# GpSimd issues its own transfers of the split w1 batches, and x is split straight from PSUM, in a three-stage fp32 kernel

## What is computed

```python
for t in range(S):                                   # linear attention with decay
    cur = einsum('bhd,bhe->bhde', u[None] * kt, vt)
    y[:, :, t] = einsum('bhd,bhde->bhe', rt, state + cur)
    state = wt[:, :, :, None] * state + einsum('bhd,bhe->bhde', kt, vt)
x = (((x @ w1) * (x @ w2)) @ w3) @ w_out             # gated layer
logits = x @ w_gate; P = exp(logits - logits.max())  # routing, 8 rounds of
for _ in range(8):                                   # normalising rows and columns
    P /= P.sum(1, keepdims=True) + 1e-09
    P /= P.sum(0, keepdims=True) + 1e-09
    P *= N / E
for e in range(E):                                   # every expert on every token
    out += P[:, e:e + 1] * (np.maximum(x @ w1[e], 0.0) @ w2[e])
```

## Time and profile before

| | |
|---|---|
| median of 3 runs | 2145.22 us (2140.44 to 2147.58) |
| the profiled execution's own time | 2151.62 us |
| its span in the profile | 2149.8 us |
| TensorE busy | 2043.4 us, 95% |
| VectorE, ScalarE, GpSimd busy | 1194.3, 816.0, 698.5 us |
| mean granted TensorE clock | 0.982 of full |
| moved by transfers | 314.92 MB, 146 GB/s over the span |

### The profile page before, as it was taken

How to read it: one execution, slowest core, us unless ns; L and a number is a source line. 1 busy time by engine, 2 the same in 40 slices (tenths; PEclk the granted TensorE clock), 3 DMA queues, 4 the chain that set the end, 5 groups by cost and what they waited for, 6 DMA issues and landing times.

```text
span 2149.8 us, 40177 instructions
## 1 busy us (share of the span) xinstructions
PE 2043.4 (95%) x16048; PEld 1695.3 (79%) x16048; DVE 1194.3 (56%) x1879; ACT 816.0 (38%) x1472; POOL 698.5 (32%) x892
## 2 busy tenths in 40 slices
PE   7799999999989789999999999999999999999998
PEld 4599889889867667777877888878877888878877
DVE  3567766675556345555575554454556445545544
ACT  4455555554433223333343333333334333333332
POOL 2566756673454764110142111011124101111111
PEclk9899999999999989999999999999999999999999
DMA  8544334431156666445454354444443444444442
GB/s 201 126 122 126 116 104 120 120 108 58 39 200 202 220 215 221 161 166 182 166 168 134 133 166 146 151 153 141 147 139 113 167 144 153 160 140 148 139 140 103
DMA packets 139529, 314.92 MB, mean 146 GB/s; under 512 B 11921, under 2 KB 77649, under 8 KB 139345
## 3 DMA queue, kind: packets, MB, share of 16 engines
q1 hardware_dynamic: 138656, 311.89, 44.7%
q10 hardware_dynamic: 688, 0.48, 0.1%
HBM read 239.87 MB, written 71.27 MB: 145 GB/s over the span
## 4 chain that ended last, share of the span: by engine, by line
PE 38%; issue 21%; POOL 2%; DVE 2%; DMA 1%; POOLq 0%; ACT 0%; SPq 0%; DVEq 0%; ACTq 0%
PE ps L1526 13%; PE ps L1528 13%; PE ps L1527 13%; POOL x L741 2%; DVE h_lo L1263 0%; DVE xs_lo L1078 0%; DMA late<-w_rows 0%; DMA Pb<-p_rows 0%; DMA w_raw<-w 0%; POOL x L779 0%; DVE tmp L1276 0%; DVE tb L1254 0%; PE ps L1620 0%; DVE tb L1258 0%; POOLq L92 0%
## 5 line engine op out<-in xcount | busy, mean ns | idle before, releaser
L741 POOL TENSOR_TENSOR x<-x,tmp 128x512 f32<-128x512 f32 x126 | 168.9, 1361 | 953.4 <-DVE tmp L1276 941.4
L1528 PE MATMUL ps<-h_hi,w 128*128 128x512 f32 x1152 | 457.6, 397 | 0.0
L1526 PE MATMUL ps<-h_hi,w 128*128 128x512 f32 x1152 | 456.6, 396 | 0.0
L1527 PE MATMUL ps<-h_lo,w 128*128 128x512 f32 x1152 | 456.5, 396 | 0.0
L819 ACT ACTIVATE tb<-ps 128x512 f32<-128x512 f32 x378 | 226.2, 598 | 509.5 <-PE ps L1528 486.6
L1014 ACT ACTIVATE h_hi<-tb 128x512 fp32r<-128x512 f32 x378 | 238.7, 632 | 451.3 <-DVE tb L1258 232.9
L1254 DVE TENSOR_TENSOR tb<-tb,ps 128x512 f32<-128x512 f32 x252 | 172.5, 686 | 289.2 <-PE ps L1528 283.4
L1263 DVE SCALAR_TENSOR_TENSOR h_lo<-tb,h_hi 128x512 fp32r<-128x512 f32 x378 | 289.3, 766 | 41.8 <-ACT h_hi L1014 35.5
L1258 DVE TENSOR_TENSOR tb<-ps,tb 128x512 f32<-128x512 f32 x252 | 173.9, 691 | 242.2 <-PE ps L1528 241.1
L1527 PEld LDWEIGHTS ps<-h_lo,w 128*128 128x128 f32 x1152 | 218.8, 190 | 51.7
L1526 PEld LDWEIGHTS ps<-h_hi,w 128*128 128x128 f32 x1152 | 217.8, 189 | 51.0
(11 more groups left out here) (154 smaller groups left out, 3181.2 us busy)
## 6 DMA issues: line engine op xcount, KB each, us to landing
early<-w_rows SPq DMA_DIRECT2D x63, 1024.0 KB, 5.6
late<-w_rows SPq DMA_DIRECT2D x63, 896.0 KB, 5.2
w<-w_rows SPq DMA_DIRECT2D x128, 384.0 KB, 4.3
w_rows<-batch SPq DMA_DIRECT2D x105, 384.0 KB, 3.2
w_rows<-w SPq DMA_DIRECT2D x64, 384.0 KB, 2.8
w_raw<-w SPq DMA_DIRECT2D x32, 576.0 KB, 4.8
Pb<-p_rows SPq DMA_DIRECT2D x24, 512.0 KB, 6.1
K<-kT SPq DMA_DIRECT2D x24, 192.0 KB, 3.7
```

The costliest lines, as they stand in the source:

```text
L741: return gp.tensor_tensor(to, a, b, ALU.add)
L1526: mm(o, w_hi, x_hi, start=start, stop=False, skip_group_check=True)
L1527: mm(o, w_hi, x_lo, start=False, stop=False, skip_group_check=True)
L1528: return mm(o, w_lo, x_hi, start=False, stop=stop, skip_group_check=True)
```

## The change

- GpSimd issues the batches' stores itself, behind each batch, and the load of the next raw w1 behind the fifth one (`make_batch`, new `load_w1` in GpSimd's program). SyncE's `keep_batch` and `load_w1` are gone, and so are SyncE's waits on `w1_made`.
- Batches begin in unit 2 (FROM_UNIT) and there are five to a unit, so 50 are made in the units. The other 55 go to the groups: four to a group, three where the y's of a later expert are added, two in group 5; the last two in group 16. In GpSimd's program of a group one batch stands ahead of the steps S4 to S6, and the others behind them.
- `xT` and GpSimd's `take_x` are gone. In slot 3 ScalarE copies all 128 rows from PSUM straight into the high plane of `yT` (256 columns) and of `x0` or `x1` (768 columns), in one instruction each where there were two. In slot 5 (was slot 6) VectorE subtracts both from PSUM into the low planes (`split_last_y`, `take_x`). Only then may SyncE issue the six moves, which carry both planes, 32 KB each. `go_up` waits for the moves (`gap_moved`) instead of for `x_split`.
- `load_early(0)`, GpSimd's and ScalarE's start on the third stage now wait for one more slice of the last unit (`up_done`, 89 instead of 88).
- The buffers of the batches are placed at the end of SBUF.

```diff
-    PER_UNIT = 6
+    FROM_UNIT, PER_UNIT = 2, 5
...
-        x_hi1 = sb("x_hi1", [P, KD, CT], f32r)
-        x_lo1 = sb("x_lo1", [P, KD, CT], f32r)
+        x1 = sb("x1", [P, 2, KD, CT], f32r)
...
-        x_hi = [sb("x_hi0", [P, KD, CT], f32r), x_hi1]
-        x_lo = [sb("x_lo0", [P, KD, CT], f32r), x_lo1]
+        x01 = [sb("x0", [P, 2, KD, CT], f32r), x1]
...
-        yT = sb("yT", [P, CT])
-        xT = sb("xT", [P, KD, CT])
...
+        yT = sb("yT", [P, 2, CT], f32r)
...
-        BEFORE = PER_UNIT * (U - 1)
-        in_unit = lambda u: range(PER_UNIT * (u - 1), PER_UNIT * u)
-        in_group = lambda G: range(min(LAST_BATCH, BEFORE + BATCHES * (G - 1)), min(LAST_BATCH, BEFORE + BATCHES * G))
+        BEFORE = PER_UNIT * (U - FROM_UNIT)
+        in_unit = lambda u: range(PER_UNIT * (u - FROM_UNIT), PER_UNIT * (u + 1 - FROM_UNIT)) if FROM_UNIT <= u < U else range(0)
...
+        per_group = lambda G: 0 if G == 0 else 2 if G == P_TURN[0] + 1 else 3 if any(y_at[n] and y_at[n][0] == G for n in range(6, Y)) else 4
+        made_before = [min(LAST_BATCH, BEFORE + sum(per_group(i) for i in range(G))) for G in range(NG + 1)]
+        in_group = lambda G: range(made_before[G], made_before[G + 1]) if G < NG else range(0)
+        assert all(BATCHES * G <= made_before[G] for G in range(1, NG))
...
-                        sp.dma_start(xT[HROW * h + HD:HROW * h + HROW, k, :],
-                                     yT[HROW * h + GAP * k:HROW * h + GAP * k + GAP, :]).then_inc(gap_moved, 16)
...
-            def load_w1(n):
-                if n:
-                    sp.wait_ge(w1_made, BATCHES * n)
-                for i, j, e, f in pieces(full_at(n)):
-                    sp.dma_start(w1_raw[:, KD * i:KD * j, :].rearrange("p (f k) c -> p f (k c)", k=KD),
-                                 w12[e, :, f:f + j - i, 0:D]).then_inc(w1_loaded, 16)
-
-            def keep_batch(x):
-                n, j = divmod(x, BATCHES)
-                sp.wait_ge(w1_made, x + 1)
-                sp.dma_start(w1_rows[n, :, :, BATCH * j:BATCH * j + BATCH, :], batch[x % 2][:, :, :, :].bitcast(f32)).then_inc(w1_kept[x % 2], 16)
-                if j == BATCHES - 1 and n + 1 < NG - 1:
-                    load_w1(n + 1)
+                        sp.dma_start(x01[u % 2][HROW * h + HD:HROW * h + HROW, :, k, :].bitcast(f32),
+                                     yT[HROW * h + GAP * k:HROW * h + GAP * k + GAP, :, :].bitcast(f32)).then_inc(gap_moved, 16)
...
-            load_w1(0)
...
-                for x in made[0:2]:
-                    keep_batch(x)
-                if u + 1 < U:
...
-                sp.wait_ge(y_copied, 2 * u)
+                sp.wait_ge(y_split, u)
+                sp.wait_ge(x_split, u)
...
-                for x in made[4:]:
-                    keep_batch(x)
...
-            sp.wait_ge(up_done, NF * (U - 1))
+            sp.wait_ge(up_done, NF * (U - 1) + 1)
...
-                made = in_group(G) if g else ()
-                for x in made[0:2]:
-                    keep_batch(x)
...
-                            for x in made[2:]:
-                                keep_batch(x)
...
-            def take_x(u):
-                pool.wait_ge(x_copied, 2 * u + 2)
-                pool.wait_ge(gap_moved, GAP_MOVE * (u + 1))
-                if u >= 2:
-                    pool.wait_ge(up_done, NF * (u - 1))
-                gp.tensor_copy(x_hi[u % 2][:, :, :], xT[:, :, :]).then_inc(x_hi_made, 1)
-                pool.wait_ge(x_hi_made, u + 1)
...
+            def load_w1(n):
+                for i, j, e, f in pieces(full_at(n)):
+                    gp.dma_start(w1_raw[:, KD * i:KD * j, :].rearrange("p (f k) c -> p f (k c)", k=KD),
+                                 w12[e, :, f:f + j - i, 0:D]).then_inc(w1_loaded, 16)
...
-            for u in range(U + 1):
-                if 1 <= u < U:
-                    for x in in_unit(u):
-                        make_batch(x)
+                gp.dma_start(w1_rows[n, :, :, BATCH * j:BATCH * j + BATCH, :], batch[x % 2][:, :, :, :].bitcast(f32)).then_inc(w1_kept[x % 2], 16)
+                if j == BATCHES - 1 and n + 1 < NG - 1:
+                    load_w1(n + 1)
+
+            for u in range(U):
+                if u == FROM_UNIT - 1:
+                    load_w1(0)
+                for x in in_unit(u):
+                    make_batch(x)
                 if u + 1 < U:
                     begin_rpad(u + 1)
-                if u:
-                    take_x(u - 1)
-                if u < U:
-                    copy_blocks(u)
-            pool.wait_ge(x_split, U)
-            pool.wait_ge(up_done, NF * (U - 1))
+                copy_blocks(u)
...
+                add_ys(S1, S4)
...
+                for x in made[0:1]:
...
-                add_ys(S3, R2)
-                for x in made[2:]:
+                add_ys(S4, R3)
+                for x in made[1:]:
                     make_batch(x)
-                add_ys(R2, NP)
...
-                for h in range(2):
-                    rows = slice(HROW * h, HROW * h + HD)
-                    copy(yT[rows, :], y_ps[rows, CT * LAST:CT * PAIRS]).then_inc(y_copied, 1)
-
-            def copy_y(u, h):
+                copy(yT[:, 0, :], y_ps[:, CT * LAST:CT * PAIRS]).then_inc(y_copied, 1)
+
+            def copy_y(u):
                 act.wait_ge(y_made, 2 * u + 2)
-                if u:
-                    act.wait_ge(x_split, u)
-                rows = slice(HROW * h, HROW * h + HD)
-                copy(xT[rows, :, :], y_ps[rows, 0:CT * LAST].rearrange("p (g t) -> p g t", t=CT)).then_inc(x_copied, 1)
+                if u >= 2:
+                    act.wait_ge(up_done, NF * (u - 1))
+                copy(x01[u % 2][:, 0, :, :], y_ps[:, 0:CT * LAST].rearrange("p (g t) -> p g t", t=CT)).then_inc(x_copied, 1)
...
-                        copy_y(u - 1, 0)
-                    if k == 4:
-                        copy_y(u - 1, 1)
+                        copy_y(u - 1)
...
-                    act.wait_ge(x_split, U)
-                    act.wait_ge(up_done, NF * (U - 1))
+                    act.wait_ge(up_done, NF * (U - 1) + 1)
...
+            def split_last_y(u):
+                dve.wait_ge(y_copied, u + 1)
+                dve.wait_ge(x_copied, u + 1)
+                low_part(yT[:, 1, :], y_ps[:, CT * LAST:CT * PAIRS], yT[:, 0, :]).then_inc(y_split, 1)
+
             def take_x(u):
-                dve.wait_ge(x_hi_made, u + 1)
-                low_part(x_lo[u % 2][:, :, :], xT[:, :, :], x_hi[u % 2][:, :, :]).then_inc(x_split, 1)
+                x = x01[u % 2]
+                low_part(x[:, 1, :, :], y_ps[:, 0:CT * LAST].rearrange("p (g t) -> p g t", t=CT), x[:, 0, :, :]).then_inc(x_split, 1)
...
-                if 1 <= u <= U and k == 6:
+                if 1 <= u <= U and k == 5:
+                    split_last_y(u - 1)
                     take_x(u - 1)
...
-                    pe.wait_ge(x_copied, 2 * u)
+                    pe.wait_ge(x_split, u)
...
-                    pe.wait_ge(x_split, u + 1)
+                    pe.wait_ge(gap_moved, GAP_MOVE * (u + 1))
...
-                                             x_hi[u % 2][:, k, :], x_lo[u % 2][:, k, :], k == 0, k == KD - 1)
+                                             x01[u % 2][:, 0, k, :], x01[u % 2][:, 1, k, :], k == 0, k == KD - 1)
...
-                    pe.wait_ge(x_copied, 2 * U)
+                    pe.wait_ge(x_split, U)
```

21 lines of the change are left out of this document (9 added, 12 removed).

## The result

The changed kernel takes 2084.99 us (median of 4 runs, 2082.86 to 2087.58) against 2146.4 us for the kernel before (the three runs told of above and a fourth): ratio 0.972, 95% interval 0.969 to 0.974, so some 61 us faster. The forecast was 2110 us and its range ended at 2087, so the gain was under-estimated.

A forecast was written before the change was run, and what follows sets the result against it. TensorE, busy for 95% of the span, was taken as the bound, so only its idle time and clock could be won. -41 + 12 - 6 = -35 us from 2145.2 gave 2110 us, range 2087 to 2137.

The forecast's parts named there:

- the circle: Groups 1 to 8: GpSimd waits for transfers that SyncE issues late, standing 147.0 us for GpSimd's batches.
- Part 1: Groups 1 to 8: SyncE no longer waits for batches; 28 us of waits and 13 of clock go, -41 us.
- the 4 us that I kept for `early` behind P: Groups 1 to 8: 4.0 of TensorE's 32.1 us of waits stay, as SyncE still waits for the turned P.
- Part 2: Groups 1 to 16: GpSimd pays for its transfers, TensorE held 10 us, clock 2 us: +12 us; units nothing.
- The price: GpSimd's time for issuing one transfer, taken at 1.1 us, between bounds of 0.52 and 3.7 us.
- The factor of two: GpSimd needs 829 ns for what VectorE does in 423, so an issue costs twice SyncE's 0.52 us.
- Part 3: Units: x's new path only moves TensorE's idle time, 17 us in all; 6 us of clock gained: -6 us.
- A: GpSimd quick enough, 0.6 us an issue, nothing held: 2098 us, or 2090 with moves landing within 2 us; chance 0.22.
- B: Units: path of x longer, each wait 3.5 us instead of 1.4: 2158 us, at half of that 2134; chance 0.09.
- C: Groups: GpSimd becomes the bound at 2.0 us an issue and the kernel slower: 2160 us; chance 0.10.
- D: SyncE stays blocked elsewhere (turned P, w2's split, products), perhaps 15 us won: 2130 us; chance 0.05.
- The signs: What the profile after should show in groups and units: waits, clock, group lengths, issues at 1.1 us.

The follow-up runs named there:

- sync_moves: The changed kernel with the transfers of w1's batches back on SyncE; new plan and new path of x stay: 2142.3 us, ratio 0.998.
- queue_alone: The kernel before with only w1's transfers issued by GpSimd; old plan of batches and old path of x stay: 2152.0 us, ratio 1.001.
- even_plan: The changed kernel with three batches in each group (two in group 5) where most had four: 2077.9 us, ratio 0.966.
- batches_alone: The kernel before with GpSimd issuing w1's transfers and the new plan of batches; x still goes the old path: 2084.9 us, ratio 0.972.
- more_adds: even_plan with two unused 128x256 additions in SBUF on GpSimd behind each batch of the units: 2096.0 us, ratio 0.975.
- more_sets: even_plan with three 128x512 memsets on GpSimd behind each batch of the units: 2087.1 us, ratio 0.971.
- late_additions: even_plan with GpSimd's additions of y put behind all of the group's batches: 2084.6 us, ratio 0.970.
- two_issues: The changed kernel with each batch's store split into two halves, 105 more issues on GpSimd: 2094.8 us, ratio 0.974.

## Why the prediction was right and wrong

**What bounds the kernel, and the circle.** Right, and shown: with SyncE's transfers back (sync_moves) the gain is gone. But I looked for the circle only in groups 1 to 8. It ran in the units too: GpSimd's idle time there was SyncE's transfers. And moving the queue alone doesn't break it (queue_alone).

**Part 1, -41 us.** Right in size: groups 1 to 8 gained 40.9 us, ScalarE's wait for raw w2 fell to 1.1 us, and the 4 us that I kept for `early` behind P stayed (3.6). Incomplete in its reason: I put all of it down to the queue. queue_alone shows that without the lighter plan GpSimd is late with y, SyncE waits 35.8 us for that, and nothing is gained.

**Part 2, +12 us.** Right in size (10 us in groups 9 to 16; the 185.0 us that I set them against ended 1.2 us before group 17 began). The price, 0.69 us and 0.30 us of waiting, 1.0 together for my 1.1, came out near by luck. The factor of two stood on `ab`, which reads PSUM; `ab_lo`, with both inputs in SBUF like GpSimd's batch, took 541 ns, which gives 0.8. The 0.30 us stood in no term, and the latencies that I set beside it are times to the first byte and not the engine's own. The mechanism is only partly mine. Waiting for GpSimd's additions took 3.3 us; the larger part is one `h_lo` held up for 6.3 us beside six additions, which no term held. even_plan removes it and gains 7 us.

**Part 3, -6 us: the step that failed.** "That is what is lost today (14.9 us and 2 in unit 1). The idle time is only moved" came out as -34.7 us at group 1's start. TensorE's waits for x (`x_lo`, and `wab_lo` behind it in unit 1) went from 23.8 us at 40 to 555 us to 5.0, where I had 17 staying 17: 18.8 us for my 0. The 1.2 GHz level went from 30.7 us in the units, worth 15.4, to none from 80 us on, for my 6. Together that is 34.2 us. Three things were wrong.
- Unit 1 was taken at 2 us. It lost some 11: a 6.9 us gap and the 1.2 GHz level from 98.1 to 111.7 us. I read the units from 150 us on.
- The waits for the moves are 5.0 us in seven units, not 17 us. In the unit of 248 to 287 us the six issues begin at 280.94, the last move lands at 286.72 and TensorE stands for 0.4 us: 7.1 us behind the level, near the 7.3 that I had costed, but TensorE comes for x only 6.7 us behind the level, the longest lead that I had allowed.
- I asked only what the path of x does in the units. GpSimd free of SyncE there, with five batches a unit from unit 2 on, which I costed at "nothing", makes x early enough on the old path as well (batches_alone). The queue without that plan doesn't: 21.2 us of waits for `x_lo` stay in queue_alone.

**Rivals.** A's number, 2090 us with the moves early, came nearest, and by luck: an issue with its wait is 1.0 us and not 0.6, and groups 9 to 16 were held. B and C did not occur: no wait for the moves over 1.5 us, 5.8 us from first issue to last landing in the unit above for B's 8, no issue near 1.8 us. C's suspicion that VectorE and GpSimd get in each other's way in SBUF was right for their operations (below), not for the issues. The Trainium skill's rule that I weighed there ("SBUF — State Buffer", section "SBUF: two separate sides": GpSimd's queue locked out by VectorE, 0.62 us growing to 3.1) isn't seen: of 105 issues the longest took 0.84 us, and from issue to landing a store took 3.7 us in the median and 8.2 at most, where SyncE's had 3.2 and 8.2. This kernel is no test of it either, with hardly an operation of the kind it names. D did not occur.

**The signs.** No wait of SyncE for a batch: so. Clock near 1.00 in the groups: 0.98. Groups 2 to 8 at 23 to 25 us: they took 23.0 to 25.6, except group 4 at 30.7. No stretch at 1.2 GHz behind the waits for the moves: so, none from 70 us to group 1. Groups 9 to 16 somewhat above 23.1 us with waits for additions: 24.5 on average, most of it group 9. Waits for the moves of 1 to 2 us in each unit: wrong, at most 1.5 in seven of them.

## What to carry to other kernels

Where two engines wait for each other in one kind of work, look for that circle in every stage that has the work, from its first appearance, and not only where the profile shows the largest wait. Moving a queue and lightening its owner's load can each be worth nothing or less and together everything, so cost a change's parts jointly, and try each alone before keeping it: here the second half could be left out. Give an engine that makes things ahead of time no more per stage than it needs to stay ahead; work done too early made the late engine's additions come in a burst.

## What the runs showed of the hardware

**VectorE against GpSimd in SBUF.** In the changed kernel at 150 to 550 us, of VectorE's 53 operations K times decay (both inputs in SBUF) the 29 with no GpSimd operation beside them took 0.68 us on average, and the 24 that had one beside them for over half their time 1.11 us (GpSimd's issues of transfers not counted). With one input in PSUM nothing changes: ab took 0.42 and 0.41 us, x's low part 0.95 and 0.95 (one and nine of them). (Worked out from the starts and ends of all of them.) The Trainium skill says this ("SBUF — State Buffer", section "Who interferes with whom"): VectorE with two SBUF inputs contends with a GpSimd instruction that reads SBUF and not with one that only writes it. The trace agrees, in more_adds and more_sets most plainly: nine K times decay that had only a memset beside them for over half their time took 0.69 us, none longer, and eleven that had only an added addition 1.80 us.

**A queue of reads keeps the other out.** I had not expected a single VectorE operation to stand through several of GpSimd's: 6.32 us beside the last five of six additions in a row, 6.17 in late_additions, 8.6 beside six multiplications in two_issues. In all traces the VectorE operations over 2.8 us in the groups lie beside two or more of GpSimd's additions of y or of these multiplications in a row, and end 0.5 us or more after the last of them. The hold-up grows with the length of that run: in the changed kernel 2.8 us beside two additions (group 14), 3.8 beside three (group 12), 6.3 beside five.

**An issue by GpSimd** costs 0.69 us for a store of 384 KB, 0.55 for one of half the size and 0.81 for a load of raw w1.
